# Attention and mixture of experts on one core: five token chunks in place of four, a deeper weight ring, half-size expert steps

## The reference

```python
# q, k, v: (4, 8, 576, 64); domain_probs (2304, 4); w1 (4, 512, 1024); w2 (4, 1024, 512); all float32
scores = (1 / sqrt(64)) * q @ k.T                        # per batch and head, 576 x 576
thresh = max(scores, -1) - tau
scores = where(scores >= thresh, scores, -1e9)
attn = exp(scores - max(scores, -1)); attn = attn / (sum(attn, -1) + 1e-9)
x = attn @ v                                             # regrouped to (2304 tokens, 512)
p = domain_probs / (sum(domain_probs, -1) + 1e-9)
for e in range(4):
    out += p[:, e:e+1] * (relu(x @ w1[e]) @ w2[e])
```

## Time and profile before

| | before |
|---|---|
| median of 3 runs | 1109.41 us (1108.31 to 1110.43) |
| the profiled execution | 1110.54 us, span 1108.7 us |
| granted TensorE clock, mean | 0.998 |
| PE busy | 1077.2 us (97%) |
| DVE, ACT, POOL busy | 603.9, 563.8, 617.8 us |
| matmuls recorded | 6556 |
| DMA | 104.40 MB, mean 94 GB/s |

### The profile page before, as it was taken

The page is one execution under the profiler, slowest core; times in us unless marked ns, Lnnn a source line. Parts: engine busy times, 40 slices in busy tenths (PEclk is TensorE's granted clock), DMA queues, the critical chain, the costliest instruction groups (busy, mean ns, idle before and its releaser), DMA issues.

```text
span 1108.7 us, 18445 instructions
## 1 busy us (share of the span) xinstructions
PE 1077.2 (97%) x6556; PEld 994.5 (90%) x6556; DVE 603.9 (54%) x1252; ACT 563.8 (51%) x1137; POOL 617.8 (56%) x768
## 2 busy tenths in 40 slices
PE   5899999999899999999999999999999999999998
PEld 4789898998798998998998989989899898989897
DVE  5877776778665675664755655645555121212121
ACT  5877675667665473563744635626445141414140
POOL 6867676768786573672844745717546152525240
PEclk9999999999999999999999999999999999999999
DMA  5533443434454241330333323304113131413121
GB/s 152 157 88 109 112 132 102 128 119 117 144 147 132 57 132 35 106 110 12 113 105 93 105 77 88 104 16 127 53 58 88 57 111 41 113 40 113 40 86 47
DMA packets 87578, 104.40 MB, mean 94 GB/s; under 512 B 40128, under 2 KB 44224, under 8 KB 87488
## 3 DMA queue, kind: packets, MB, share of 16 engines
q1 hardware_dynamic: 87184, 102.90, 32.2%
q10 hardware_dynamic: 304, 0.33, 0.1%
HBM read 98.47 MB, written 4.72 MB: 93 GB/s over the span
## 4 chain that ended last, share of the span: by engine, by line
PE 91%; DVE 2%; POOL 2%; ACT 1%; DMA 1%; issue 1%; SPq 0%; ACTq 0%; DVEq 0%
PE e_ps L857 12%; PE e_ps L859 12%; PE e_ps L843 12%; PE e_ps L858 12%; PE e_ps L845 12%; PE e_ps L844 12%; PE t_ps L789 6%; PE s_ps L777 3%; PE x_ps L816 3%; PE s_ps L778 3%; PE x_ps L818 3%; PE x_ps L801 1%; POOL w_lo L755 1%; DMA k_raw<-kT 1%; DVE p L989 1%
## 5 line engine op out<-in xcount | busy, mean ns | idle before, releaser
L755 POOL TENSOR_TENSOR w_lo<-stage,w_hi 128x512 fp32r<-128x512 f32 x240 | 313.3, 1310 | 198.3 <-ACT w_hi L946 195.1
L843 PE MATMUL e_ps<-x_hi,w_hi 128*128 128x320 f32 (+1 forms) x896 | 285.9, 319 | 1.5 <-DVE h_lo L1027 1.4
L845 PE MATMUL e_ps<-x_hi,w_lo 128*128 128x320 f32 (+1 forms) x896 | 280.8, 313 | 0.0
L844 PE MATMUL e_ps<-x_lo,w_hi 128*128 128x320 f32 (+1 forms) x896 | 280.7, 313 | 0.0
L946 ACT ACTIVATE w_hi<-stage 128x512 fp32r<-128x512 f32 x256 | 157.7, 624 | 143.4 <-PE e_ps L859 106.8
L857 PE MATMUL e_ps<-w_hi,h_hi 128*128 128x512 f32 x576 | 228.2, 396 | 0.0
L859 PE MATMUL e_ps<-w_hi,h_lo 128*128 128x512 f32 x576 | 225.4, 391 | 0.0
L858 PE MATMUL e_ps<-w_lo,h_hi 128*128 128x512 f32 x576 | 224.6, 390 | 0.0
L1027 DVE SCALAR_TENSOR_TENSOR h_lo<-e_ps,h_hi 128x320 fp32r<-128x320 f32 (+1 forms) x224 | 111.6, 499 | 123.9 <-ACT h_hi L936 122.2
L843 PEld LDWEIGHTS e_ps<-x_hi,w_hi 128*128 128x128 f32 x896 | 168.9, 189 | 3.0 <-DVE h_lo L1027 2.7
L844 PEld LDWEIGHTS e_ps<-x_lo,w_hi 128*128 128x128 f32 x896 | 169.0, 189 | 0.3
(11 more groups left out here) (63 smaller groups left out, 1472.8 us busy)
## 6 DMA issues: line engine op xcount, KB each, us to landing
stage<-w SPq DMA_DIRECT2D x256, 256.0 KB, 2.8
k_raw<-kT SPq DMA_DIRECT2D x94, 144.0 KB, 2.8
v_raw<-v SPq DMA_DIRECT2D x40, 128.0 KB, 2.1
out<-acc SPq DMA_DIRECT2D x18, 256.0 KB, 2.0
q_raw<-qT SPq DMA_DIRECT2D x32, 144.0 KB, 2.9
q_raw<-qT SPq DMA_DIRECT2D x16, 112.0 KB, 2.7
q_raw<-qT SPq DMA_DIRECT2D x16, 96.0 KB, 2.6
v_raw<-v SPq DMA_DIRECT2D x80, 16.0 KB, 2.1
```

Source lines behind the costliest of these rows:

```text
L755: gp.tensor_tensor(w_lo[:, m % RING, :], stage[:, m % STAGES, :], w_hi[:, m % RING, :], ALU.subtract).then_inc(s_wl, 1)
L843: mm(ps[:, 0:n], w_hi[:, piece, tile], x_hi[:, k, cols], start=k == 0, stop=False)
L844: mm(ps[:, 0:n], w_hi[:, piece, tile], x_lo[:, k, cols], start=False, stop=False)
L845: op = mm(ps[:, 0:n], w_lo[:, piece, tile], x_hi[:, k, cols], start=False, stop=k == KT - 1)
```

## The change

The chunks become 384, 512, 384, 512, 512 tokens: five instead of four, so all weights are loaded and split five times (320 pieces). No chunk is wider than 512, so an up group is one group of 384 or 512 columns. `x_hi` and `x_lo` become a ring of 1408 columns in which a pair of heads can wrap (then its copy is made by two instructions). The attention heads of batch 1 are cut at 320 and 256 query rows instead of 448 and 128, which changes the widths of the `pv` parts. The weight ring has 14 slots and 4 staging slots. DVE makes the low part of every fourth piece in chunk 0 and of every second in the last chunk (48 pieces; POOL 272). Each up and each down step on PE has 6 matmuls instead of 12. The reciprocal is written over the sum, and some small tiles share memory. All constants of the order are new. Units woven in: 32 in chunk 0, 52 in chunk 1, 36 in chunk 2, none in chunks 3 and 4.

```diff
-RING = 12
-STAGES = 3
+RING = 14
+STAGES = 4
-CHUNKS = ((384, 0, 0), (640, 704, 384), (640, 0, 1024), (640, 640, 1664))
-X_COLS = 1344
+X_COLS = 1408
+X_FIRST = 128
+CHUNKS = tuple((n, (X_FIRST + first) % X_COLS, first)
+               for n, first in ((384, 0), (512, 384), (384, 896), (512, 1280), (512, 1792)))
 VISITS = ((0, 0, 0, 384, (0, 0, 0, 0)),
-          (1, 0, 384, 192, (0, 384, 0, 384)), (1, 1, 0, 448, (0, 128, 512, 640)),
-          (2, 1, 448, 128, (256, 512, 0, 512)), (2, 2, 0, 576, (0, 384, 0, 384)),
+          (1, 0, 384, 192, (0, 384, 0, 384)), (1, 1, 0, 320, (0, 0, 0, 0)),
+          (2, 1, 320, 256, (0, 512, 256, 0)), (2, 2, 0, 576, (0, 384, 0, 384)),
           (3, 3, 0, 576, (0, 384, 0, 384)))
-DVE_TO = E * PIECES
+DVE_FROM = (len(CHUNKS) - 1) * E * PIECES
...
-        self.x_col = CHUNKS[c][1] + self.token - CHUNKS[c][2]
+        col = (X_FIRST + self.token) % X_COLS
+        whole = min(n, X_COLS - col)
+        self.x_cols = [(col, 0, whole)] + ([(0, whole, n - whole)] if whole < n else [])
...
 def lo_on_dve(m):
-    return m < DVE_TO and m % 4 == 2
+    return m % 4 == 2 if m < E * PIECES else m >= DVE_FROM and m % 2 == 0
...
-PLAN = dict(first=3.52, period=3.24, experts=14.84, end=12.59, weights=26.12, weight=6.89, prob=20.73)
+PLAN = dict(first=-1.79, period=2.89, experts=16.98, end=13.3, weights=31.7, weight=8.16, prob=21.1)
...
-                todo.append((mm(12, g.cols[1]), "up", g))
+                todo += [(mm(6, g.cols[1]), "up", g, part) for part in range(2)]
-                todo += [(mm(12, D), "down", g, half) for half in range(2)]
+                todo += [(mm(6, D), "down", g, part) for part in range(4)]
...
-                        for k in range(KT):
+                        for k in range(x[1] * KT // 2, (x[1] + 1) * KT // 2):
...
-                        op.then_inc(s_up, 1)
+                        if x[1] == 1:
+                            op.then_inc(s_up, 1)
...
-                        for f in range(x[1] * FT // 2, (x[1] + 1) * FT // 2):
+                        for f in range(x[1] * FT // 4, (x[1] + 1) * FT // 4):
...
-                        if x[1] == 1:
+                        if x[1] == 3:
                             op.then_inc(s_dn, 1)
...
-                    ve.reciprocal(col(inv, u), col(total, u)).then_inc(s_rec, 1)
+                    ve.reciprocal(col(total, u), col(total, u)).then_inc(s_rec, 1)
```

More of the change, by code:

```diff
@@ L24 @@
 PIECES = 2 * FT
-RING = 12
-STAGES = 3
+RING = 14
+STAGES = 4
 SCALE = HD ** -0.5
 EPS = 1e-9
-CHUNKS = ((384, 0, 0), (640, 704, 384), (640, 0, 1024), (640, 640, 1664))
-X_COLS = 1344
+X_COLS = 1408
+X_FIRST = 128
+CHUNKS = tuple((n, (X_FIRST + first) % X_COLS, first)
+               for n, first in ((384, 0), (512, 384), (384, 896), (512, 1280), (512, 1792)))
+WIDEST = 512
 VISITS = ((0, 0, 0, 384, (0, 0, 0, 0)),
[2 rows of a table removed]
[2 rows of a table added]
           (3, 3, 0, 576, (0, 384, 0, 384)))
 PT_COLS = 768
-DVE_TO = E * PIECES
+DVE_FROM = (len(CHUNKS) - 1) * E * PIECES
 EARLY = 3
@@ L200, in ups_through @@
     return (UPS_TO[t - 1] if t else 0) + (f + 1) * len(col_parts(CHUNKS[t // E][0]))
[L206 to L211, removed]
-PLAN = dict(first=3.52, period=3.24, experts=14.84, end=12.59, weights=26.12, weight=6.89, prob=20.73)
+ALONE = dict(load=-4.8, q_hi=8.39, q_lo=12.4, k_hi=0.51, k_lo=-8.08, v_hi=8.36, v_lo=-1.65, max=9.17, thr=11.83,
+             exp=7.51, mask=6.84, eps=8.04, rec=0.42, norm=20.48, tr=-2.41, phi=5.82, plo=7.84, pv=13.77, xo=17.62,
+             xs=10.27, x_hi=4.88, x_lo=7.99)
+AMONG = dict(load=-9.57, q_hi=1.94, q_lo=1.96, k_hi=-3.03, k_lo=-7.62, v_hi=-2.41, v_lo=5.96, max=-1.29, thr=-1.0,
+             exp=8.31, mask=2.72, eps=1.37, rec=6.04, norm=-1.68, tr=10.24, phi=7.34, plo=7.7, pv=12.16, xo=6.29,
+             xs=15.65, x_hi=9.79, x_lo=9.94)
+PLAN = dict(first=-1.79, period=2.89, experts=16.98, end=13.3, weights=31.7, weight=8.16, prob=21.1)
 def halves_of(u):
@@ L293, in timeline @@
             g = x[0]
-            if name == "up":
+            if name == "up" and x[1] == 1:
                 add(t + 0.1, "hhi", g)
@@ L297, in timeline @@
                 up_end[g.t, g.j] = t
-            elif x[1] == 1:
+            elif x[1] == 3:
                 add(t + 0.1, "acc", g)
@@ L325 @@
              k_lo=1.45, v_lo=0.9, thr=0.22, eps=0.22, norm=1.1, wlo=1.32,
-             pv32=1.1, down=2.75, k_hi=0.68, v_hi=0.47, exp=0.75, whi=0.63,
+             pv32=1.1, down=1.37, k_hi=0.68, v_hi=0.47, exp=0.75, whi=0.63,
              max=0.76, mask=0.9, rec=0.17, acc=0.76, wlo_dve=0.93, prob=3.6)
@@ L344, in takes @@
     if name == "up":
-        return mm(12, x.cols[1])
+        return mm(6, x.cols[1])
     if name == "pv":
@@ L409, in follows @@
     if name == "x_hi":
-        return [("xs", x.parts[-1])] + ([("up", UP_GROUPS[UPS_TO[(x.c - 1) * E - 1] - 1])] if x.c >= 2 else [])
+        return [("xs", x.parts[-1])] + ([("up", UP_GROUPS[UPS_TO[(x.c - 1) * E - 1] - 1], 1)] if x.c >= 2 else [])
     if name == "x_lo":
@@ L419, in follows @@
         elif i < FT:
-            room = [("up", UP_GROUPS[ups_through(t, i) - 1])]
+            room = [("up", UP_GROUPS[ups_through(t, i) - 1], 1)]
         else:
-            room = [("down", DOWN_GROUPS[DOWNS_TO[t] - 1], 1)]
+            room = [("down", DOWN_GROUPS[DOWNS_TO[t] - 1], 3)]
         return [("w_load", x)] + room
@@ L429, in follows @@
     if name == "hhi":
-        return [("up", x)]
+        return [("up", x, 1)]
     if name == "hlo":
@@ L434, in follows @@
         first = CHUNKS[x.c][2] // P
-        return [("down", x, 1), ("prob", 0)] + ([("store", STORE_GROUPS[first - 1])] if x.e == 0 and x.c else [])
+        return [("down", x, 3), ("prob", 0)] + ([("store", STORE_GROUPS[first - 1])] if x.e == 0 and x.c else [])
     return [("acc", x)]
@@ L458, in settle @@
         name = step[0]
[L459 to L469, removed]
+        if name in ("up", "down") and step[2]:
+            before = [(name, step[1], step[2] - 1)]
+        elif name == "down":
+            before = [last_step(step[1].before)]
         else:
             before = [b for b in follows(*step) if b in due]
+        if name == "down" and step[1].j == 0:
+            g, part = step[1:]
+            before.append(("hlo", UP_GROUPS[UPS_TO[g.t] - 1]))
+            before += [low(g.t * PIECES + FT + part * FT // 4 + f) for f in range(2)]
         kind = "down" if name == "up" else name
@@ L535, in build @@
         x_sum = sb("x_sum", [P, SEQ])
+        dp_in = x_sum[:, 0:TT * E].rearrange("p (t e) -> p t e", e=E)
+        dp_sum = x_sum[:, TT * E:TT * (E + 1)]
+        warm = x_sum[:, SEQ - 1:SEQ]
         x_hi = sb("x_hi", [P, KT, X_COLS], F32R)
@@ L544, in build @@
             p.append(p2)
-        h_hi = sb("h_hi", [P, FT, 640], F32R)
-        h_lo = sb("h_lo", [P, FT, 640], F32R)
-        acc = sb("acc", [P, 5, D])
+        h_hi = sb("h_hi", [P, FT, WIDEST], F32R)
+        h_lo = sb("h_lo", [P, FT, WIDEST], F32R)
+        acc = sb("acc", [P, WIDEST // P, D])
         ident = sb("ident", [P, P])
-        dp_in = sb("dp_in", [P, TT, E])
-        dp_sum = sb("dp_sum", [P, TT])
         prob = sb("prob", [P, E, TT])
[L552 to L557, removed]
+        small = sb("small", [P, 4, 4])
+        tau_col, neg_m, thr, total = (small[:, i, :] for i in range(4))
         s_ps = ctx.enter_context(nc.psum_tensor("s_ps", [P, 2, 512], F32))
@@ L741, in _ @@
                     if u >= SOLID:
-                        gp.tensor_scalar(twin, tail, col(inv, u), 1.0, ALU.mult, ALU.mult).then_inc(s_twin, 1)
+                        gp.tensor_scalar(twin, tail, col(total, u), 1.0, ALU.mult, ALU.mult).then_inc(s_twin, 1)
                         pool.wait_ge(s_twin, u - SOLID + 1)
-                    gp.tensor_scalar(tile, tile, col(inv, u), 1.0, ALU.mult, ALU.mult
+                    gp.tensor_scalar(tile, tile, col(total, u), 1.0, ALU.mult, ALU.mult
                                      ).then_inc(s_norm, 1)
@@ L748, in _ @@
                     pool.wait_ge(s_xh, pair.index + 1)
-                    c0 = pair.x_col
-                    gp.tensor_tensor(x_lo[:, pair.k, c0:c0 + pair.n], x_sum[:, 0:pair.n],
-                                     x_hi[:, pair.k, c0:c0 + pair.n], ALU.subtract).then_inc(s_xl, 1)
+                    for c0, first, n in pair.x_cols:
+                        op = gp.tensor_tensor(x_lo[:, pair.k, c0:c0 + n], x_sum[:, first:first + n],
+                                              x_hi[:, pair.k, c0:c0 + n], ALU.subtract)
+                    op.then_inc(s_xl, 1)
                 elif name == "wlo":
@@ L822, in _ @@
                     ps = e_ps[:, g.bank, :]
-                    if name == "up" or x[1] == 0:
+                    if x[1] == 0:
                         if g.before is None:
@@ L831, in _ @@
                         f, (c0, n) = g.j, g.cols
-                        if c0 == 0:
+                        if c0 == 0 and x[1] == 0:
```

(18 more changed lines are left out.)

## The result

The changed kernel takes 1098.49 us (median of 4 runs, 1096.14 to 1100.8) against 1109.92 in the same comparisons: ratio 0.9896, 95% interval 0.9882 to 0.9911, so 11.4 us or 1.0% faster. The forecast was 1098.9.

What follows compares the result with a forecast made beforehand. PE's matmuls, number times distance, were taken to bound the kernel from 301 us on. Terms -10.1 - 5.0 + 1.3 + 3.3 = -10.5 us took 1110.54 to 1100.0, or 1098.9 us as median; range 1089 to 1108 us.

Steps and rivals of the forecast that it cites:

- Fewer up matmuls: Expert up matmuls on PE: 768 fewer for the same columns, 338.0 us becoming 327.9, -10.1 us.
- Attention passes: The pv passes of batch 1 on PE: the new cut at 320 and 256 rows saves 5.0 us.
- Weights covered: 64 more weight pieces on DMA, ACT, POOL and DVE: covered by PE's own work, so 0 us.
- First phase: Before the experts: 14 pieces instead of 12 ahead of the first expert step, +1.3 us, middle of 0 and 2.6.
- Waits in the woven part: PE's waits in chunks 0 to 2, where attention is woven in: 11.2 us against 7.9 before, +3.3 us.
- The working of the waits: Chunks 0 to 2: waits judged from POOL's load, forecast at 71%, 71% and 76% against 72%, 59% and 52% before.
- Half-size steps: I take 0: Steps of 6 matmuls on PE: no cost in PE's rate, 0 us; any gain counted in the waits.
- The slower rival: Woven part: POOL makes PE late, 4 us per up stretch, 1123.7 us; decides from 21.7 us of waits; chance 0.05.

Runs made afterwards that it cites:

- split256: Changed kernel with each 512-wide up matmul made as two of 256 in the same bank, 1152 more matmuls; 1110.34 us.
- nodve_last: Changed kernel with all low parts of the last chunk on POOL, none on DVE; 1097.23 us, ratio 0.9886 to the kernel before.
- stages3: Changed kernel with 3 staging slots instead of 4, weight ring still 14; 1110.22 us, ratio 1.0 to the kernel before.
- control: The changed kernel run again with no edit; 1098.89 us, ratio 0.99 to the kernel before.
- dve_mid: Changed kernel with every fourth low part of chunks 1 and 2 on DVE instead of POOL; 1107.18 us, ratio 0.9976 to the kernel before.
- mix: Changed kernel with the order constants of before for the first phase alone, new ones for the woven part; 1102.87 us.
- oldconst: Changed kernel with its order made from the three lines of constants of the kernel before; 1103.85 us, ratio 0.9952 to the kernel before.
- b_steps6: Kernel before, four chunks, with its up and down steps cut in two and nothing else changed; 1113.38 us, ratio 1.0037.
- steps12: Changed kernel with only the half-size steps undone, up and down steps of 12 matmuls; 1149.99 us, ratio 1.0362 to the kernel before.

## Why the prediction was right

**The sum against the two profiled executions.** Cut at the first expert matmul (87.0 and 88.2 us), the difference of the two spans, -14.3 us, is +1.3 in the first phase, -12.4 in what PE is busy for behind it, and -3.2 in its waits (8.0 to 4.8 us). The forecast had +1.3, -15.1 (matmuls and attention passes) and +3.3, in all -10.5.

**Fewer up matmuls, -10.1 us: right where experts run alone.** 174.1 us for a 512 chunk was forecast and is there to the tenth; split256 prices a matmul at 13.5 ns by itself.

**Attention passes, -5.0 us: right.** No run isolates them, but the two traces do: the `pv` matmuls fell from 540 to 504, and their distances from start to start, idle time left out, add up to 72.0 us before and 67.1 after, -4.9.

**Weights covered, 0: right in the chunks without attention.** Chunks 3 and 4 have no idle PE, and nodve_last doesn't change that. In the woven chunks it hangs on the fourth staging slot (stages3).

**First phase, +1.3 us: right in size, and no more than that.** The first expert matmul moved from 87.0 to 88.2 us. Five profiles with the same lists up to there (the changed kernel, control, split256, dve_mid, nodve_last) have it between 87.8 and 89.8, a spread larger than the term. With the old constants it comes at 87.1 (mix, oldconst), which points to the constants, and not only the two pieces.

**Waits in the woven part, +3.3 us (11.2 in all): the mis-sized term.** PE idles for 4.8 us there, 6.4 less than forecast; the control has 6.0. On the other side, PE's work fell by 2.7 us less than the 15.1 of the sum. The prediction's own chunks say as much: 190.6 + 265.6 + 192.6 + 2 x 174.1 against the 205.9 + 300.2 + 282.0 + 221.4 of the earlier trace rows is -12.5, and not -15.1. That the forecast meets the median to 0.4 us is partly luck: these two errors are opposite in sign, and the profiled execution that the sum started from lay above all four of the timed runs of before, while that of after was the fastest of its four (the executions differ by 14.4 us, the medians by 11.4).

**The working of the waits was wrong too.** It scaled them with POOL's load, 71, 71 and 76%. POOL's load came out at 75, 71 and 76% (145.6 / 194.7, 188.4 / 264.9, 147.7 / 194.8), so it did not fall, but PE waited least for POOL, and dve_mid took POOL work away and lost 8.3 us.

**"Half-size steps: I take 0."** Not borne out, in PE's rate or in what they give. In the kernel before they cost PE 3.3 us of busy time for the same matmuls (b_steps6), which is about the size of the 2.7 us that are missing above; that it is the same cost was not isolated in five chunks. What they give in five chunks is 51 us: the steps, the fourth staging slot and the constants are worth 51, about 11 and 5 us, each undone by itself, and without the first, this change would have been 3.6% slower than the kernel before. The slower rival named POOL and 21.7 us of waits; the real danger is attention that is left over behind a chunk's expert work and then runs alone (in steps12's chunk 1, POOL's p ends 9.4 of PE's 24.5 us of waits). The list could have shown it before any run: count the units between the last down of chunk 1 and the first up of chunk 2.

## What to carry to other kernels

When an engine has no gaps, count its instructions: here each matmul cost 13.3 to 13.5 ns beside its columns, and 768 fewer outweighed 16.8 MB more of weights. Their load and rounding were hidden where PE had no other work than experts; beside attention they were hidden only with a fourth staging slot. When the background work of a chunk grows against the foreground, the grain of the foreground decides whether the background finishes in time; try it both ways, for half was right here, a quarter cost 19 us and the whole 51, while in the kernel before half cost 3.7. A load average doesn't forecast waits.

## What was not expected

Moving 32 small operations from POOL to DVE cost 8.3 us, though POOL is the busier one over the whole span (661.6 against 630.8 us): in chunk 1 it is not, and there PE waits for DVE. A list with 20% more matmuls (split256) gave back a quarter of its price in waits and late starts elsewhere. And in and just behind the thinly filled first phase a profiled execution has between no dip (split256, oldconst) and two dips (control, nodve_last) to 1.2 GHz, each at a granted clock of 0.5 where it is deepest, beside a spread of 4.7 us between executions.
